# Two 64-column products of a chunked recurrence merged into one product with 128 weight columns

## What is computed

```python
for t in range(S):
    y[:, :, t] = np.einsum('bhd,bhde->bhe', rt, state)
    Sa = np.einsum('bhde,bhe->bhd', state, at)
    state_decay = state * wt[:, :, None, :] - np.einsum('bhd,bhe->bhde', Sa, bt)
    state = state_decay + np.einsum('bhd,bhe->bhde', vt, kt)
# then
h = np.maximum(x @ w_in, 0.0)
out1 = h * sigmoid(conv3(h)) @ w_out
# then, for each expert e: softmax(causal(scale * q k^T)) @ v @ wo[e], weighted by the gate
```

## Time and profile before

| | |
|---|---|
| median of 3 runs | 918.24 us (911.47 to 920.96) |
| the profiled execution | 923.58 us, of which the span of instructions is 921.9 us |
| TensorE (matmuls) busy | 824.6 us, 89% |
| VectorE busy | 559.7 us, 61% |
| ScalarE busy | 317.4 us, 34% |
| GpSimd busy | 259.5 us, 28% (nearly all of it in the first 367 us) |
| mean granted TensorE clock | 0.946 of full |

### The profile page before, as it was taken

The page is one execution under the profiler, slowest core; times in us unless marked ns, Lnnn a source line. Parts: engine busy times, 40 slices in busy tenths (PEclk is TensorE's granted clock), DMA queues, the critical chain, the costliest instruction groups (busy, mean ns, idle before and its releaser), DMA issues.

```text
span 921.9 us, 27713 instructions
## 1 busy us (share of the span) xinstructions
PE 824.6 (89%) x11872; PEld 597.0 (65%) x11872; DVE 559.7 (61%) x1235; ACT 317.4 (34%) x741; POOL 259.5 (28%) x525
## 2 busy tenths in 40 slices
PE   3428989998999988889998999988999998999988
PEld 3428889988998988864465654545644656545555
DVE  8995795878599742136528645357464277354474
ACT  4102331323133232222227542246432266322364
POOL 2087777778778877000000000000000000000000
PEclk9999895979599798899999999999999979999999
DMA  3645575657566574620100000100001000000000
GB/s 117 153 85 122 126 163 113 134 139 140 122 157 138 113 158 102 157 78 26 44 1 15 16 15 1 43 0 23 15 8 43 1 8 22 16 1 0 1 15 30
DMA packets 130922, 61.33 MB, mean 67 GB/s; under 512 B 106544, under 2 KB 119792, under 8 KB 130800
## 3 DMA queue, kind: packets, MB, share of 16 engines
q1 hardware_dynamic: 96156, 32.61, 16.3%
q10 hardware_dynamic: 34644, 26.95, 11.3%
HBM read 45.37 MB, written 14.16 MB: 65 GB/s over the span
## 4 chain that ended last, share of the span: by engine, by line
PE 75%; DVE 11%; issue 5%; ACT 5%; POOL 2%; DMA 1%; SPq 0%; ACTq 0%; DVEq 0%
PE ps_all L808 8%; PE ps_all L792 8%; PE ps_scan L105 5%; PE ps_all L852 5%; PE ps_scan L188 4%; PE ps_all L918 4%; PE ps_all L900 4%; PE ps_all L930 4%; PE ps_scan L130 3%; PE ps_scan L167 3%; PE ps_all L795 3%; PE ps_all L802 2%; PE ps_all L835 2%; PE ps_scan L122 2%; PE ps_scan L114 2%
## 5 line engine op out<-in xcount | busy, mean ns | idle before, releaser
L328 POOL TENSOR_TENSOR t_update<-solver_then_w_down 128x133 f32<-128x133 f32 (+13 forms) x251 | 118.6, 473 | 88.1 <-DMA solver_then_w_down<-l_blocks 39.1
L330 POOL TENSOR_TENSOR solver_then_w_down<-solver_then_w_down,t_update 128x133 f32<-128x133 f32 (+13 forms) x251 | 132.7, 529 | 19.7
L105 PE MATMUL ps_scan<-decayed_a_and_eye,scaled_then_x 40*128 40x104 f32 x768 | 67.6, 345 | 46.5 <-DVE decayed_a_and_eye L362 45.2
L1129 DVE TENSOR_REDUCE minus_max<-ps_all 128x1 f32<-128x128 f32 (+5 forms) x96 | 55.3, 617 | 66.8 <-PE ps_all L904 66.8
L105 PEld LDWEIGHTS ps_scan<-decayed_a_and_eye,scaled_then_x 40*128 40x128 f32 x768 | 62.8, 252 | 48.6 <-issue 47.7
L808 PE MATMUL ps_all<-gated,solver_then_w_down 128*128 128x384 f32 x256 | 91.1, 499 | 0.0
L792 PE MATMUL ps_all<-scaled_then_x,inputs_then_w_up 128*128 128x384 f32 x256 | 88.8, 490 | 1.8 <-ACT ak_l_then_ffn L970 1.8
L1028 ACT ACTIVATE probs_t<-ps_all 128x512 f32<-128x512 f32 (+3 forms) x128 | 55.1, 452 | 69.9 <-PE ps_all L918 69.3
L808 PEld LDWEIGHTS ps_all<-gated,solver_then_w_down 128*128 128x128 f32 x256 | 46.0, 189 | 44.6 <-issue 19.1
L792 PEld LDWEIGHTS ps_all<-scaled_then_x,inputs_then_w_up 128*128 128x128 f32 x256 | 47.6, 190 | 36.3 <-ACT ak_l_then_ffn L970 6.0
L232 ACT ACTIVATE x_rhs<-ps_scan 128x320 f32<-128x320 f32 x48 | 21.0, 438 | 141.3 <-PE ps_scan L122 70.5
(11 more groups left out here) (117 smaller groups left out, 1523.8 us busy)
## 6 DMA issues: line engine op xcount, KB each, us to landing
r_t_and_v_t<-in_rv ACTq DMA_DIRECT2D x48, 160.0 KB
inputs_then_w_up<-in_x ACTq DMA_DIRECT2D x46, 160.0 KB
solver_then_w_down<-l_blocks SPq DMA_DIRECT2D x22, 256.0 KB, 4.6
uv_and_ruv<-in_v ACTq DMA_DIRECT2D x48, 80.0 KB, 3.7
y_t<-y_out SPq DMA_DIRECT2D x24, 160.0 KB
out<-out_rows SPq DMA_DIRECT2D x24, 160.0 KB, 1.8
inputs_then_w_up<-in_x ACTq DMA_DIRECT2D x46, 81.4 KB
inputs_then_w_up<-in_x ACTq DMA_DIRECT2D x46, 80.0 KB
```

Of the source, the lines that this page charges most:

```text
L105: last = nc.tensor.matmul(PS[:, o:o + ROWS], weights, AL[c % NK][rows(h), p, :], start=True, stop=True)
L328: return (lambda: eng.tensor_tensor(tmp[:, 0:cols, 0:rest], l[:, s:s + 1, s + 1:BLK].broadcast_to(shape), t[:, 0:cols, s:s + 1].broadcast_ ...
L330: lambda: eng.tensor_tensor(t[:, 0:cols, s + 1:BLK], t[:, 0:cols, s + 1:BLK], tmp[:, 0:cols, 0:rest], ALU.subtract))
L1129: nc.vector.tensor_reduce(NM[:, v:v + 1], PS[:, first_bank(v) * 512:first_bank(v) * 512 + n], AX.X, ALU.min).then_inc(m["nm"], 1)
```

## The change

r, v and u of a step are put into one buffer `VUR` with the order v, u, r (`[ROWS, P8, 3, C]`) for each pair; the layout in DRAM has for half 0 the order v, u, r and for half 1 the order r, u, v, with zeros where u will be written. So v and u of a head stand side by side, in the order in which their products lie in PSUM, and one matmul takes both as 128 weight columns. `uv_r` becomes 16 products of 128 weight columns instead of 32 of 64. The load of r and v also carries the zeros: 6 KB instead of 4 KB for each partition. ACT writes u into the loaded buffer with a stride; it already waited for that load.

```diff
-    RV = [sb(f"r_t_and_v_t{n}", [ROWS, 2, P8, C]) for n in range(3)]
-    RT = [RV[n][:, 0, :, :] for n in range(3)]
-    VT = [RV[n][:, 1, :, :] for n in range(3)]
+    VUR = [sb(f"v_t_u_t_r_t{n}", [ROWS, P8, 3, C]) for n in range(3)]
+    RT = lambda n, h: VUR[n][rows(h), :, 2 - 2 * h, :]
+    UT = [VUR[n][:, :, 1, :] for n in range(3)]
...
-    UT = sb("u_t", [ROWS, P8, C])
...
             pe.wait_ge(m["ut_sb"], n + 1)
             for p in range(P8):
                 for h in range(2):
-                    nc.tensor.matmul(PH[h][own(h), seg(p, C)], VT[n % 3][rows(h), p, :], RT[n % 3][rows(h), p, :],
-                                     start=True, stop=True)
-                for h in range(2):
-                    last = nc.tensor.matmul(PH[h][own(1 - h), seg(p, C)], UT[rows(h), p, :], RT[n % 3][rows(h), p, :],
+                    last = nc.tensor.matmul(PH[h][:, seg(p, C)], VUR[n % 3][rows(h), p, h:h + 2, :].rearrange("r k t -> r (k t)"), RT(n % 3, h)[:, p, :],
                                             start=True, stop=True)
             last.then_inc(m["h"], 1)
...
-                act.dma_start(RV[n % 3][rows(h), :, :, :].rearrange("r k p t -> r (k p t)"),
-                              in_rv[n, h].rearrange("r k p t -> r (k p t)")).then_inc(m[f"r{n % 3}"], 16)
+                act.dma_start(VUR[n % 3][rows(h), :, :, :].rearrange("r p k t -> r (p k t)"),
+                              in_rv[n, h].rearrange("r p k t -> r (p k t)")).then_inc(m[f"r{n % 3}"], 16)
...
-                nc.scalar.activation(UT[:, :, :], by8(PU, C)[0:ROWS], ACT.Copy, scale=-1.0).then_inc(m["ut_sb"], 1)
+                nc.scalar.activation(UT[n % 3], by8(PU, C)[0:ROWS], ACT.Copy, scale=-1.0).then_inc(m["ut_sb"], 1)
```

More of the change, by code:

```diff
@@ L176, in out_from_state @@
                     o = place(6, p) + D
-                    nc.tensor.matmul(PS[rows(h), o:o + C], STT[n % 2][rows(h), p, :], RT[n % 3][rows(h), p, :],
+                    nc.tensor.matmul(PS[rows(h), o:o + C], STT[n % 2][rows(h), p, :], RT(n % 3, h)[:, p, :],
                                      start=(p % 4 == 0), stop=False, skip_group_check=True)
@@ L1295, in lay_out @@
     vn = v.reshape(NPAR, P8, 2, NCH, C, D).transpose(3, 0, 2, 4, 1, 5).reshape(NT, 2, C, P8, D)
+    rs, vs = split(r), split(v)
+    vur = np.zeros((NT, 2, D, P8, 3, C), np.float32)
+    vur[:, 0, :, :, 0], vur[:, 0, :, :, 2] = vs[:, 0], rs[:, 0]
+    vur[:, 1, :, :, 0], vur[:, 1, :, :, 2] = rs[:, 1], vs[:, 1]
     return {"in_x": x, "in_v": np.ascontiguousarray(vn),
-            "in_rv": np.ascontiguousarray(np.stack([split(r), split(v)], 3))}
+            "in_rv": vur}
 def kernel(r, k, v, w, a, b, moe_w_in, moe_conv_w, moe_w_out, moe2_w_gate, moe2_wq, moe2_wk, moe2_wv, moe2_wo):
```

## The result

The changed kernel takes 961.54 us (median of 4 runs, 951.99 to 964.46); the kernel before, on the same chip, takes 919.6 us (911.47 to 922.18). The ratio is 1.0454, with a 95% interval of 1.0354 to 1.0554. It is slower, and above the upper end of the forecast range. (In three comparisons further down, of e3_idle, e10_after_pad and e11_wide96, the executions spread by 2 to 3%, so their whole spread is given, and the ratio of the last holds for its quickest executions alone.)

A forecast was written before the change was run, and what follows sets the result against it. TensorE, busy 89% of the span, was taken as the bound. Longer groups +27.6, filled waits -10, instruction waits -4 and solver -4 gave +9.6 us: 928 us on the 918.24 us median, range 908 to 944.

The forecast's parts named there:

- The group: Merged product on TensorE: 2.1 us instead of 0.99 at full clock, 3.85 instead of 2.15 at half; +27.6 us in all.
- The filled waits: TensorE's idle time before L122 and inside the old group, which the longer group would fill: -10 us.
- instruction waits: TensorE's waits at L195 and L148 for instructions not yet there: a third or more would go, -4 us (bounds 0 and -10.8).
- The solver's slack: In steps 14 to 20 TensorE is ahead of GpSimd's block inverses, so added time there is absorbed: -4 us (bounds 0, -8).
- The rest costs nothing: Load of r and v grown from 160 to 240 KB, copy of u and VectorE's masking would add no time.
- near 0.87: Sign to look for: TensorE's mean granted clock over 60 to 405 us, the recurrence, would stay near 0.87.
- rival C: More half clock from fewer moving columns: two or three further stretches, 5 to 10 us each, giving 945 us; chance 0.12.
- In the trace the drops follow waits, and this change has fewer of them: The argument given against more half clock on TensorE: clock drops come after waits, which the change would reduce.
- half-clock stretches changed by more than 15 us: Sign that the forecast is wrong: the sum of TensorE's half-clock stretches changes by more than 15 us.

The follow-up runs named there:

- e3_idle: Kernel before, with eighteen waits for long-past events put ahead of L122 on TensorE in each step: 941.64 us, ratio 1.0352.
- e10_after_pad: Changed kernel, merged group left at 64 moving columns, more moving columns in the products beside it (L129, L163, L104): 959.76 us, before 919.28.
- e11_wide96: Changed kernel with 96 moving columns in the merged group instead of 64: 928.96 us; ratio 1.0015 by the four quickest executions, 1.01 by the means of all.
- e6_load: Kernel before, its load grown by 384 zeros for each partition (220 KB a transfer instead of 160): 925.52 us, ratio 1.0106.
- e1_layout: Changed kernel's buffer, DRAM layout, larger load and strided copy of u, but the 64-column products of the kernel before: 929.16 us, ratio 1.0195.
- e12: Repeat on another chip of the new layout and larger load with the kernel before's 64-column products: 930.38 us, ratio 1.0134.
- e5: The changed kernel itself, unaltered, measured again on another chip: 956.09 us, ratio 1.0437 to the kernel before.
- e15: Changed kernel (64 moving columns), r and v loaded without zeros in two transfers a half, issued at the end of ACT's step: 976.59 us, ratio 1.0621.
- e2: Changed kernel with 128 moving columns instead of 64 in the merged products of seven of eight pairs: 932.31 us, ratio 1.0211.
- e13: Changed kernel with 128 moving columns, r and v loaded without zeros in two transfers a half at the end of ACT's step: 927.28 us, ratio 1.0106.
- e14: Changed kernel with 128 moving columns, full 240 KB load with zeros, issued at the end of ACT's step: 934.8 us, ratio 1.0185.
- e16: Kernel before, with only its load of r and v moved to the end of ACT's step: 927.65 us, ratio 1.0094.
- e8: Changed kernel with 128 moving columns, r and v loaded without zeros in three transfers a half, issued early: 934.88 us, ratio 1.0162.
- e4_pad: Kernel before, with more moving columns in L130, L167 (64 for 40) and L105 (128 for 104): 912.79 us, ratio 1.003.
- e7_shift: Kernel before, with 64 more instructions (semaphore waits) on TensorE ahead of its first step: 925.8 us in one run, before 914.94.

## Why the prediction was wrong, by its steps

**The group, 2.1 us at full clock and 3.85 at half: right.** It takes 1.93 us and 0.1 for the step, and 3.6 us at half clock (from 242.69 to L121 at 246.29 us). Only the 1.93 us lie a little under the forecast 2.0 to 2.1. A row with the same weight shape and other moving columns was enough. The page "TensorEngine Tiling (Array Packing)" of the Trainium skill, section "Key Properties", says that tiles can load weights and multiply in parallel; the rows agree, since four records in four quadrants took 58 ns where two records of 128 weight columns take 120 (1.93 us over 16 pairs).

**The filled waits, -10, and instruction waits, -4: right in kind, too small together.** The "issue" waits fell from 18.3 to 4.2 us. Nearly all went, not a third of those at L195 and L148; the count of instruction transfers went from 94 to 88. The runs don't show why the remaining blocks are so seldom late; that a slower stream gives each more time is still only argued.

**The solver's slack, -4: not shown.** ACT's waits for block inverses are gone, which agrees, but GpSimd now waits 64.8 us for VectorE (30.1 before) and no longer sets the pace:

```profile
POOL t_update L324 <- DVE solver_then_w_down L326: 64.8, 9, 16.7
```

**"The rest costs nothing": failed.** The larger load was priced by who waits for it, and nobody does. It costs 1.1% at three quarters of its growth (e6_load) and 1.3 to 2.0% with the layout around it (e1_layout and its repeat). That it does so by making instruction blocks late is argued, from L122's wait of 10.3 to 14.5 us against 5.4, and not shown. In the changed kernel itself those blocks hardly wait, so its part there can't be read from a wait.

**The clock: the step that failed.** The sum has no term for the clock, and the signs to look for had it "near 0.87"; that term measured 33 us. Half clock was left to rival C, at 0.12, and C is the case that came about. The sentence that failed is "In the trace the drops follow waits, and this change has fewer of them". It is true of the nine falls of before. I took what they had in common for what a fall needs. The change made a new kind of stretch, whose like no fall of before could show. The doubt was in the prediction (the group keeps the array's columns moving for half the time) and I tied it to a wait that it didn't need. C was also too small: "two or three" further stretches against five more and 66.6 us in all, and I had counted 71.6 us of half clock before, in five stretches, where nine sum to 88.6 and the stretch up to the first rise comes on top. The prediction's own sign, half-clock stretches changed by more than 15 us, told it rightly. The page "TensorE: Matmul & The Clock Gate" of the Trainium skill, section "HAM oscillation", likewise looks for idle gaps; the rows around 167 us have none, so here the measurement decides against taking that as the only cause.

**Sizes.** The change costs 4.4 to 4.5%. How much of a kernel's loss is the clock can be estimated from the result of every execution: the span times one minus its mean clock is the time lost to half clock, and the rest is what would be left at full clock. (It counts the stretch ahead of the first rise as full clock, which for the change with its late rise puts some 10 us into the wrong column, and it takes waits within half clock as if they shrank too.) Means over the executions, us:

| kernel | lost to half clock | the rest |
|---|---|---|
| before, on three chips | 36 to 39 | 876 to 877 |
| layout alone (e1, e12) | 53, 52 | 874, 878 |
| the change (first runs, e5) | 79, 79 | 880, 876 |
| e15 (64 columns) | 99 | 876 |
| 128 columns (e2, e13, e14) | 38, 38, 39 | 891, 889, 892 |
| 96 columns (e11) | 36 | 889 |
| e6 (larger load), e16 (late load) | 47, 45 | 877, 879 |

By this estimate nearly the whole loss of the change and of the layout alone is in the clock. With the clock held, the merged group is not free: the kernels with 96 and 128 columns lose no more to the clock than the kernel before and still take 12 to 15 us more, which is their 1 to 2%. The layout's 1.3 to 2.0% and e2's 2.1% look alike and are different things, so they can't be added up to the change's 4.5%.

**What stays open.** What it is in e1, e6 and e16 that lowers the clock: all their falls follow waits, but the traces were compared with one of before that is itself among its slower executions. What the strided copy of u costs by itself: no run had it alone. Why L113 waits about 5 us for v at about 360 us in the change, e5, e2 and e15, and not in e8 and e11: the load is issued at 354.95 and transfers of `w_in` on SP's queue, 512 and 256 KB each, are in flight then, which argues for contention, but no run took it away. Why e15 lost more than the change did. No version was faster than the kernel before: the best are e4_pad (1.003) and the quick runs of e11_wide96.

## What to carry to other kernels

Merging small products into one with more weight columns saves instructions and not time where the quadrants already ran side by side: compare the start-to-start times of rows with the same weight shape first. Price a product also by what it leaves TensorE's clock: here a group of 128 weight and 64 moving columns ran without a pause and was followed by half clock, and one kernel's trace shows this only if it already has such a group. A transfer that nobody waits for may still have a price (1.1% in e6_load): don't set it to nothing because no wait names it.

## What the runs showed of the hardware

- The clock fell from 2.4 to 1.2 GHz with no wait of TensorE in the 4 us ahead, 2.9 to 3.8 us behind the start of a group of 32 records with 128 weight and 64 moving columns, in 10 of 14 falls; with 128 moving columns in the same number of instructions in none of 5. Half clock behind the first rise was 136.1 us against 71.7 us.
- Those added moving columns cost the group no time: 1.93 us with 64 and with 128.
- In fp32, 16 products of 128 weight columns took 1.93 us at full and 3.60 us at half clock. The page "TensorE: Matmul & The Clock Gate" of the Trainium skill, section "LDWEIGHTS (loading the stationary operand)", gives a time by the number of weight columns with no clock in it; the rows show the group's time nearly doubling with half clock.
- TensorE's waits for instructions stood at one place of a block of 256 of its records (15 of 16 waits), and 64 instructions more in front moved them by 64 (17 of 17, e7_shift).
- Sixty more KB in each load, read by nobody, took the kernel up by 1.1%, at a mean clock of 0.945 to 0.953 against 0.951 to 0.970.
